# The diagonal of a linear attention by row products and the matrix engine, and the last output tile stored by thirds

## The chip, the cores and the metric

The kernel runs on one core of a Trainium2 chip. The metric is the time of one execution on the device in microseconds, lower is better. A core has a matrix engine (TensorE, PE in the rows; its weight loads are PEld), a vector engine (DVE), a scalar engine (ACT), GpSimd (POOL) and a sync engine (SP) that here only issues transfers. Each engine works through its own instructions in order and waits on semaphores. All numbers are float32 or its rounded form fp32r.

## What is computed

Three stages: a linear attention with decay over 4 sequences of 768 tokens and 8 heads of 48 features, then two feed-forward blocks over the 3072 tokens. The change is in how the first stage's diagonal term is made, and in how the last result is stored.

```python
for t in range(S):                                     # S = 768, head_dim D = 48
    cur = einsum('bhd,bhe->bhde', u * k[t], v[t])      # the diagonal term: token t sees itself, weighted by u
    y[t] = einsum('bhd,bhde->bhe', r[t], state + cur)
    state = w * state + einsum('bhd,bhe->bhde', k[t], v[t])
h = x @ w_in;  x = (max(h, 0) + alpha * min(h, 0)) @ w_out      # 384 -> 2048 -> 384
h = x @ w_in2; x = (h * tanh(softplus(h))) @ w_out2             # 384 -> 2048 -> 384
```

The diagonal term needs one number for each token and head: the sum over d of u[h, d] * r[t, h, d] * k[t, h, d].

## The kernel before

Tokens are cut into 24 chunks of 128. A chunk's attention is two units (four heads, or two pairs of heads, each); unit v belongs to chunk v // 2. For a unit, scaled keys and queries are made by POOL and DVE (`scale_key_level`, L320, and `scale_query_level`, L310), PE makes the scores level by level (`score`, L1092), ACT first writes the diagonal into `scores` (`fill_diagonal`, L865, an identity scaled by the token's number) and then copies the high levels over it (`copy_high`, L877), DVE picks the low levels under a mask (`pick_scores`, L605), and PE multiplies by the values (`attend`, L1118). `sum_state` (L1070) makes the state that the next chunk sees; ACT copies it out of PSUM (L863).

The feed-forward blocks take tiles of 512 tokens. Up and down products run over 16 steps (`up`, L1031, `down`, L1052); each step is nine matmuls of 512 columns, because weights and activations are split into a high and a low part. The attention of chunks 5 to 23 is spread over the steps of the first block. Chunks 0 to 4 have nothing to be hidden behind: this is the attention-only stage (`first_tile` of each engine), from the start to about 62 us. There PE also runs `warm` matmuls (L1021), which multiply the identity by itself into `acc[2]`. After unit 9 three more follow, and then the first `up`, which needs all that chunks 0 to 3 left in `x_parts`.

The inputs r and k arrive twice: `rk_rows` (from `rk_t`, one head feature in a partition, four pairs of heads by 128 tokens along the free axis; `load_rows`, L343) and `rkv_tok` (from `rkv`, one token in a partition, 384 features; `load_rk`, L351). The diagonal of a chunk is made from the latter: POOL multiplies r by k (`products`, L482), then by u (L486), DVE sums each head's 48 features (`sum_diagonal`, L629), and ACT's `fill_diagonal` waits for that at the chunk's first unit. In POOL's order of the stage a chunk has queries of unit 0, `rows_for_state` (L469) of the chunk before, `scale_for_state` (L496), queries of unit 1, `rows_for_state`, and `products` of the next chunk. After chunk 4 POOL splits weight slot 0 (L475).

SP issues, in its own order: decay, u (`bonus_tok`), rows, r and k, v of chunks 0 and 1, then for each chunk c its rows (which wait for the scores and state rows that still use the buffer), r and k of chunk c + 1, the holes of chunk c - 3 and v. Six heads' outputs fill 96 of 128 partitions of `x_parts`; the other two heads are copied into the holes by six small transfers for each chunk (`fill_holes`, L330). Of chunk 3's six, ACT issues three and SP three; SP's stand behind `load_weights(3)`, which waits for POOL's split of slot 0.

The last output tile: PE ends its last step, ACT copies the three banks `acc[0..2]` scaled by 2 (`copy_out`, L847) and issues one store of 768 KB.

## Time and profile before

| | |
|---|---|
| three timed runs, us | 980.93, 983.01, 983.13; median 983.01 |
| profiled execution, us | 983.2, of which the profile's span is 981.4 |
| busy share of the span | PE 98%, DVE 68%, ACT 63%, POOL 38% |
| PE busy by 40th of the span | 6 9 8 9, then 9 to the end, last 7 |
| granted PE clock by 40th | 7, then 9 |

Times in rows are microseconds from the span's start. "Idle before" and the name behind the arrow tell how long an engine had nothing in work and what let it go on; "issue" is time for which the profile shows no wait. The granted clock is 1.00 at 2.4 GHz and 0.50 at 1.2 GHz. PE's matmuls are pipelined and their ends modelled, so the distance from one start to the next is the better measure there.

### The profile page before, as it was taken

What the parts mean: (1) busy time and instruction counts of PE and PEld (TensorE: products, weight loads), DVE (VectorE), ACT (ScalarE), POOL (GpSimd) and SP (SyncE); (2) the same over time, 40 slices, a digit from 0 to 9 for tenths busy, and PEclk for the clock granted to TensorE, in tenths of its full rate; (3) what the DMA queues carried; (4) which work ended last, traced back from release to release, by engine and by line L of the source; (5) the groups of instructions that cost most, each with busy time, mean ns of one, the idle gap of its engine ahead of it and who ended that gap; (6) DMA issues with size and microseconds to landing.
All of it is one profiled execution on the core that took longest, in us unless ns stands there. A gap on an engine that the chain in (4) does not pass through costs nothing.

```text
span 981.4 us, 24146 instructions
## 1 busy us (share of the span) xinstructions
PE 964.2 (98%) x9568; PEld 786.5 (80%) x9568; DVE 664.7 (68%) x1384; ACT 622.7 (63%) x1285; POOL 373.2 (38%) x664
## 2 busy tenths in 40 slices
PE   6989999999999999999999999999999999999997
PEld 5668787888888888888888888888888888888886
DVE  7997776666666666556653437867777777677775
ACT  7766545454544455555445658878777777787775
POOL 8988787666666676666501430000000000000000
PEclk7999999999999999999999999999999999999999
DMA  6353322212211121111004230100001000000000
GB/s 187 100 151 107 111 64 78 56 49 59 78 48 59 48 78 45 46 54 55 15 10 173 97 115 33 33 12 21 33 33 33 0 32 0 22 10 1 33 0 33
DMA packets 22309, 54.33 MB, mean 55 GB/s; under 512 B 4928, under 2 KB 10432, under 8 KB 22208
## 3 DMA queue, kind: packets, MB, share of 16 engines
q1 hardware_dynamic: 20384, 43.43, 14.8%
q10 hardware_dynamic: 1824, 9.49, 2.4%
q8 instruction: 71, 1.16, 0.5%
q14 instruction: 30, 0.25, 0.1%
HBM read 41.10 MB, written 9.44 MB: 51 GB/s over the span
## 4 chain that ended last, share of the span: by engine, by line
PE 93%; POOL 5%; issue 1%; DMA 0%; ACT 0%; SPq 0%; POOLq 0%; ACTq 0%
PE acc L1063 41%; PE hid L1047 30%; PE lev L1047 10%; PE lev L1114 7%; POOL arena L317 2%; PE tok L1131 2%; PE tok L1137 2%; PE tok L1088 1%; POOL arena L469 1%; POOL ruk L482 1%; POOL arena L496 0%; POOL mask L448 0%; POOL ruk L486 0%; DMA x_parts<-y 0%; POOL w_lo L475 0%
## 5 line engine op out<-in xcount | busy, mean ns | idle before, releaser
L1047 PE MATMUL hid<-x_parts,w_hi 128*128 128x512 f32 x864 | 290.1, 390 | 1.6 <-DMA x_parts<-y 1.6
L1063 PE MATMUL acc<-g_hi,w_hi 128*128 128x512 f32 x576 | 231.3, 402 | 1.4 <-issue 1.4
L1063 PE MATMUL acc<-g_hi,w_lo 128*128 128x512 f32 x576 | 225.4, 391 | 0.0
L1047 PEld LDWEIGHTS hid<-x_parts,w_hi 128*128 128x128 f32 x864 | 162.4, 188 | 37.0 <-issue 2.7
L622 DVE COPY_PREDICATED scores<-mask,lev 64x128 f32<-64x128 int8 x420 | 149.9, 357 | 30.5 <-ACT scores L886 18.6
L1047 PE MATMUL hid<-x_parts,w_lo 128*128 128x512 f32 x432 | 168.3, 390 | 0.0
L1063 PE MATMUL acc<-g_lo,w_hi 128*128 128x512 f32 x576 | 163.0, 391 | 0.0
L931 ACT ACTIVATE relu_neg<-hid 128x512 f32<-128x512 f32 x96 | 57.2, 596 | 160.8 <-PE hid L1047 158.9
L709 DVE SCALAR_TENSOR_TENSOR hid<-relu_neg,neg_slope,hid 128x512 f32<-128x512 f32 x96 | 72.5, 755 | 124.7 <-ACT hid L932 124.3
L1063 PEld LDWEIGHTS acc<-g_hi,w_hi 128*128 128x128 f32 x576 | 108.2, 188 | 25.6 <-issue 2.0
L1063 PEld LDWEIGHTS acc<-g_lo,w_hi 128*128 128x128 f32 x576 | 108.5, 188 | 23.4 <-issue 0.3
L1063 PEld LDWEIGHTS acc<-g_hi,w_lo 128*128 128x128 f32 x576 | 108.3, 188 | 21.1
L317 POOL TENSOR_TENSOR arena<-arena,power 112x128 f32<-112x128 f32 x282 | 114.4, 440 | 18.3 <-DVE w_lo L703 18.3
L758 DVE SCALAR_TENSOR_TENSOR arena<-arena 128x512 f32<-128x512 f32 x96 | 66.4, 692 | 52.1 <-ACT arena L971 52.1
L845 ACT ACTIVATE g_hi<-hid 128x512 fp32r<-128x512 f32 x96 | 57.4, 598 | 68.5 <-DVE hid L709 67.7
L327 POOL TENSOR_TENSOR arena<-arena,power_rev 112x128 f32<-112x128 f32 x228 | 94.0, 447 | 16.3 <-PE lev L1114 15.0
L469 POOL TENSOR_TENSOR arena<-arena,power_split 112x512 f32<-112x512 f32 x46 | 58.7, 1277 | 99.9 <-PE tok L1137 99.9
L1047 PE MATMUL lev<-x_parts,w_hi 128*128 128x512 f32 x288 | 96.3, 389 | 0.0
L1047 PEld LDWEIGHTS hid<-x_parts,w_lo 128*128 128x128 f32 x432 | 81.2, 188 | 17.1
L693 DVE TENSOR_TENSOR g_lo<-hid,g_hi 128x512 fp32r<-128x512 f32 x96 | 66.2, 690 | 39.4 <-ACT g_hi L845 39.3
L1114 PEld LDWEIGHTS lev<-arena 48*64 48x64 f32 x4472 | 75.0, 136 | 11.1 <-issue 8.9
L1114 PE MATMUL lev<-arena 48*64 48x32 f32 (+1 forms) x4472 | 79.7, 223 | 2.5 <-DVE arena L317 1.8
(101 smaller groups left out, 1353.1 us busy)
## 6 DMA issues: line engine op xcount, KB each, us to landing
w_raw<-weights SPq DMA_DIRECT2D x32, 384.0 KB, 3.5
arena<-rk_t SPq DMA_DIRECT2D x48, 192.0 KB, 3.6
arena<-rkv SPq DMA_DIRECT2D x24, 384.0 KB, 3.2
arena<-rkv SPq DMA_DIRECT2D x24, 192.0 KB, 2.6
x_dram<-result ACTq DMA_DIRECT2D x6, 768.0 KB, 4.1
arena<-x_dram SPq DMA_DIRECT2D x6, 768.0 KB, 4.4
out<-result ACTq DMA_DIRECT2D x6, 768.0 KB, 3.3
x_parts<-y SPq DMA_DIRECT2D x141, 16.0 KB, 1.9
```

What stands on the lines that cost most here:

```text
L317: return engine.tensor_tensor(dst, src, spread(table[0:ROWS, pairs, 0:m], 2, CHUNK // (2 * m)), ALU.mult)
L327: return engine.tensor_tensor(dst, src, spread(table[0:ROWS, pairs, HALF - m:HALF], 2, CHUNK // (2 * m)), ALU.mult)
L469: nc.gpsimd.tensor_tensor(r_state[0:ROWS, x], spread(rk_rows[0:ROWS, par, 0, pairs], 1, 2), power_split[0:ROWS, :, pairs], ALU.mult).then_ ...
L622: nc.vector.copy_predicated(dst, pick, src).then_inc(pick_done if done < 2 * low_levels(rep) - 1 else mask_done, 1)
L693: nc.vector.tensor_tensor(g_lo[:, j % RING], hid[j % 2][:, 0:TILE], g_hi[:, j % RING].bitcast(F32), ALU.subtract).then_inc(glo_done, 1)
L709: nc.vector.scalar_tensor_tensor(hid[j % 2][:, 0:TILE], relu_neg[:, j % 2], neg_slope[:, j:j + 1], hid[j % 2][:, 0:TILE], ALU.mult, ALU.ad ...
L758: nc.vector.scalar_tensor_tensor(root[:, d], eps[:, d], 0.75, seed[:, d], ALU.add, ALU.mult).then_inc(root_done, 1)
L845: nc.scalar.activation(g_hi[:, j % RING], hid[j % 2][:, 0:TILE], ACT.Copy).then_inc(ghi_done, 1)
L931: nc.scalar.activation(relu_neg[:, j % 2], hid[j % 2][:, 0:TILE], ACT.Relu, scale=-1.0)
L1047: last = nc.tensor.matmul(to[:, 0:TILE], w[:, j, kt * P:(kt + 1) * P], x[:, par, kt], start=x is x_hi and w is w_hi and kt == 0, stop=x is ...
L1063: last = nc.tensor.matmul(acc[d][:, 0:TILE], w[:, j, cols], g[:, j % RING], start=j == 0 and g is g_hi and w is w_hi, stop=j == STEPS - 1 ...
L1114: last = nc.tensor.matmul(level_scores(banks, l)[tokens, 2 * q + u], k[rows, tokens], t[rows, wanted], start=True, stop=True)
```

## The change

For chunks 0 to 4 the diagonal is made in another way. POOL multiplies r by k once, in the row layout, into `rk_prod` (112 partitions by 512, double buffered in the memory of `relu_neg`, which this stage doesn't use). PE multiplies that by `u_rows`, a small new input that holds u in the columns of its head: for each of the four pairs of heads one matmul with the 112 by 128 product as weights and two columns moving, into the first eight columns of `acc[2]`. ACT copies these into `diag`. DVE's reduction goes for these chunks. From chunk 5 on all is as it was. The `warm` matmuls, which write the same bank, now wait for ACT's copy. The order on PE: chunk 0's diagonal ahead of unit 0's scores, the next chunk's behind each odd unit's `warm`.

The wide load of u moves from the head of SP's order to behind `load_weights(2)`; the small one stands behind the rows of chunk 0. r is no longer loaded by token for chunks 0 to 4.

At the end, the last down step runs output third by output third, three matmuls each, instead of all high parts and then all low parts. ACT copies and stores thirds 0 and 2, DVE copies third 1 and SP stores it: three stores of 256 KB.

```diff
+        rk_prod = relu_neg.rearrange("p r (a t) -> p r a t", a=PAIRS)
+        by_token = CHUNKS_PER_TILE + 1
# SP
             def load_rk(c):
-                reached(sp, s_rk, c - 1)
+                reached(sp, s_rk, c - 1 - by_token)
                 reached(sp, kstate_done, c - 1)
-                sp.dma_start(rkv_tok[:, c % 2, 0:2], rkv[c, :, 0:2]).then_inc(rk_in[c % 2], 16)
+                first = 0 if c >= by_token else 1
+                sp.dma_start(rkv_tok[:, c % 2, first:2], rkv[c, :, first:2]).then_inc(rk_in[c % 2], 16)
...
-            sp.dma_start(bonus_tok[:], bonus.partition_broadcast(P)).then_inc(s_bonus, 16)
             sp.wait_ge(zero_pool, 1)
             load_rows(0)
+            sp.dma_start(u_rows[0:ROWS], bonus_rows).then_inc(u_in, 16)
...
                 if c == 2:
                     load_weights(2)
+                    sp.dma_start(bonus_tok[:], bonus.partition_broadcast(P)).then_inc(s_bonus, 16)
...
-            sp.wait_ge(stored, 16 * 2 * TILES)
+            sp.wait_ge(last_copied[1], 1)
+            sp.dma_start(out[TILES - 1][:, 1], result[:, 1]).then_inc(stored, 16)
+            sp.wait_ge(stored, 16 * (2 * TILES - 1 + KT))
# POOL
+            def product_by_row(c):
+
+                pool.wait_ge(rows_in[c % 2], 32 * (c // 2 + 1))
+                reached(pool, diag_done, c - 1)
+                nc.gpsimd.tensor_tensor(rk_prod[0:ROWS, c % 2], rk_rows[0:ROWS, c % 2, 0], rk_rows[0:ROWS, c % 2, 1],
+                                        ALU.mult).then_inc(prod_in, 1)
...
-                products(1, 1, 1)
+                product_by_row(1)
...
-                    products(c + 1, 1 - par, (c + 1) // 2 + 1)
+                    if c + 1 < by_token:
+                        product_by_row(c + 1)
+                    else:
+                        products(c + 1, 1 - par, (c + 1) // 2 + 1)
...
-            products(0, 0, 1)
+            product_by_row(0)
# DVE
-                sum_diagonal(0, 0)
...
-                        sum_diagonal(c + 1, (c + 1) % 2)
+                        if c + 1 == by_token:
+                            sum_diagonal(c + 1, (c + 1) % 2)
...
+            dve.wait_ge(stored, 16 * (2 * TILES - 1))
+            dve.wait_ge(last_product, 2)
+            nc.vector.tensor_scalar(result[:, 1], acc[1][:, 0:TILE], 2.0, 0.0, ALU.mult, ALU.add).then_inc(last_copied[1], 1)
# ACT
+            def copy_diagonal(c):
+
+                act.wait_ge(diag_done, c + 1)
+                nc.scalar.activation(diag[:, c % 2], acc[2][:, 0:H], ACT.Copy).then_inc(s_diag, 1)
...
                     if x == 0:
+                        copy_diagonal(c)
                         fill_diagonal(v)
...
-            copy_out(2 * TILES - 1, out[TILES - 1], 2.0)
+            m = 2 * TILES - 1
+            act.wait_ge(stored, 16 * m)
+            for d in (0, 2):
+                act.wait_ge(last_product, d + 1)
+                nc.scalar.activation(result[:, d], acc[d][:, 0:TILE], ACT.Copy, scale=2.0).then_inc(last_copied[d], 1)
+                act.wait_ge(last_copied[d], 1)
+                act.dma_start(out[TILES - 1][:, d], result[:, d]).then_inc(stored, 16)
# PE
+            def diagonal(c):
+
+                pe.wait_ge(prod_in, c + 1)
+                reached(pe, s_diag, c)
+                for p in range(PAIRS):
+                    last = nc.tensor.matmul(acc[2][:, 2 * p:2 * p + 2], rk_prod[0:ROWS, c % 2, p], u_rows[0:ROWS, p],
+                                            start=True, stop=True)
+                last.then_inc(diag_done, 1)
...
+                pe.wait_ge(u_in, 16)
+                diagonal(0)
                 pe.wait_ge(zero_act, 1)
...
                     if PER_CHUNK <= v < FIRST - 1:
+                        pe.wait_ge(s_diag, v // PER_CHUNK + 1)
                         warm(acc[2])
+                    if v % PER_CHUNK and v < FIRST - 1:
+                        diagonal(v // PER_CHUNK + 1)
...
-            for j in range(STEPS - LAG2, STEPS):
+            for j in range(STEPS - LAG2, STEPS - 1):
                 down2(2 * TILES - 1, (TILES - 1) * STEPS + j, j)
+
+            j = STEPS - 1
+            pe.wait_ge(ghi2_done, TILES * STEPS)
+            pe.wait_ge(glo2_done, TILES * STEPS)
+            for d in range(KT):
+                cols = slice(KT * P + d * P, KT * P + (d + 1) * P)
+                for w, g in ((w_hi, g_hi), (w_lo, g_hi), (w_hi, g_lo)):
+                    last = nc.tensor.matmul(acc[d][:, 0:TILE], w[:, j, cols], g[:, j % RING], start=False, stop=g is g_lo)
+                last.then_inc(last_product, 1)
```

## Rows read from the trace of the kernel before

**Rows 1.** The chain that ended last, around the first up: start, duration, what.

```profile
56.13 1.84 POOL w_lo L475
...
58.48 3.31 DMA x_parts<-y
...
61.92 2.31 PE hid L1047 x9
```

**Rows 2.** Timeline of POOL: start, duration, line and instruction, idle before.

```profile
3.57 4.04 POOL L448 TENSOR_SCALAR_AFFINE_SELECT mask<-mask 128x64 int8<-128x64 int8 x10
9.12 1.00 POOL L482 TENSOR_TENSOR ruk<-arena 128x384 f32<-128x384 f32 x1 [1.51 <-DMA arena<-rkv]
...
11.16 2.41 POOL L317 TENSOR_TENSOR arena<-arena,power 112x128 f32<-112x128 f32 x6
...
33.66 1.01 POOL L482 TENSOR_TENSOR ruk<-arena 128x384 f32<-128x384 f32 x1
...
35.70 2.43 POOL L317 TENSOR_TENSOR arena<-arena,power 112x128 f32<-112x128 f32 x6
...
42.66 1.28 POOL L469 TENSOR_TENSOR arena<-arena,power_split 112x512 f32<-112x512 f32 x1
43.88 1.01 POOL L482 TENSOR_TENSOR ruk<-arena 128x384 f32<-128x384 f32 x1
```

**Rows 3.** Timeline of DVE, first pick and a whole chunk.

```profile
15.27 3.15 DVE L622 COPY_PREDICATED scores<-mask,lev 64x128 f32<-64x128 int8 x8 [1.11 <-ACT scores L886]
...
40.82 0.54 DVE L629 TENSOR_REDUCE diag<-ruk 128x8 f32<-128x384 f32 x1
41.28 3.17 DVE L622 COPY_PREDICATED scores<-mask,hid 64x128 f32<-64x128 int8 x8
...
50.73 0.54 DVE L629 TENSOR_REDUCE diag<-ruk 128x8 f32<-128x384 f32 x1
```

**Rows 4.** Timeline of PE in the stage: transposes, warm, units 0 to 4, unit 6.

```profile
7.09 0.65 PE L1028 MATMUL acc<-ident,power_rev 128*128 128x128 f32 x4 [0.49 <-DVE w_pow L587]
7.58 1.46 PE L1021 MATMUL acc<-ident 128*128 128x512 f32 x4
10.82 1.82 PE L1114 MATMUL lev<-arena 48*64 48x64 f32 x104 [1.78 <-DVE arena L317]
13.72 3.20 PE L1114 MATMUL hid<-arena 48*64 48x64 f32 x104 [1.08 <-POOL arena L317]
...
19.59 3.20 PE L1114 MATMUL lev<-arena 48*64 48x64 f32 x104
...
27.50 1.82 PE L1114 MATMUL hid<-arena 48*64 48x64 f32 x104
...
31.32 1.82 PE L1114 MATMUL lev<-arena 48*64 48x64 f32 x104
...
40.34 1.83 PE L1114 MATMUL lev<-arena 48*64 48x64 f32 x104 [0.23 <-issue]
```

**Rows 5.** PE in the windows of the clock's fall and rise: length, busy (count), granted clock, DMA.

```profile
13.00:14.00 1.00, 0.28 (x10) 0.82 0.18 48
...
27.00:28.00 1.00, 1.00 (x42) 0.85 0.00 0
```

**Rows 6.** Weight loads of `warm` on PE: ns min/median/max, first and last start.

```profile
L1021 PEld LDWEIGHTS acc<-ident x22: 186/189/337, 3.7 to 53.2; 128*128 128x128 f32 x22
```

**Rows 7.** Timeline of ACT, the first fill of the diagonal.

```profile
11.88 1.28 ACT L874 ACTIVATE scores<-ident,diag 128x128 f32<-128x128 f32 x4 [1.85 <-DVE diag L629]
```

**Rows 8.** The chain at the end: the copies ahead of the last store.

```profile
976.11 1.57 ACT result L855 x3
```

**Rows 9.** The page's list of transfers: KB each, median us from issue to landing.

```profile
arena<-rkv SPq DMA_DIRECT2D x24, 192.0 KB, 2.6
...
out<-result ACTq DMA_DIRECT2D x6, 768.0 KB, 3.3
```

**Rows 10.** Timeline of PE in the first block, where it once stood still.

```profile
119.23 0.63 PE L1063 MATMUL acc<-g_hi,w_hi 128*128 128x512 f32 x1 [1.37 <-issue]
```

23 lines of the change are left out of this document (18 added, 5 removed).

## The prediction

> **What bounds the kernel now.** The page says 98% PE, and from the first `up` at 61.92 to the last product PE hardly stops. The change touches only what lies ahead of that and the last store, so I read four things: who releases the first `up`, what the engines of the attention-only stage do, at what clock PE runs there, and the tail.
>
> The chain of waits at the first `up` reads backwards: the last holes, issued from 58.48, landed 3.31 later; ahead of them in SP's order is the load of weight slot 3, which waited for POOL's split of slot 0 (56.13 + 1.84) [rows 1]. Behind that stands POOL's order of the stage, without a pause from 9.12 on. One chunk on POOL lasts from 33.66 to 43.88, that is 10.2 us (its products start on the same beat; the reduction on DVE, 40.82 to 50.73, has a beat of 9.9) [rows 2, 3]. PE's beat of a whole chunk, unit 4 to unit 6, is 40.34 - 31.32 = 9.02 us, 0.23 of it a wait, so 8.8 of work [rows 4]. So three engines lie within 1.4 us of each other: whoever takes work off POOL and DVE and puts it on PE has to ask PE first.
>
> In its early part the stage runs at two clocks. The granted clock falls from 1.00 to 0.50 within 13 to 14 and is back within 27 to 28 [rows 5]; a unit's scores last 3.20 us in between and 1.82 outside [rows 4]. Before the fall PE had done one unit and nothing else since the warm matmuls ended at 9.04, with pauses of 1.78 and 1.08 [rows 4].
>
> **POOL.** For a chunk the two products take 35.70 - 33.66 = 2.04 us; the row product has 112 by 512 elements like `rows_for_state`, 1.28 by its row [rows 2]. It saves 0.76 for each of chunks 0 to 4. Chunk 0's also starts when the masks end (3.57 + 4.04 = 7.61) and not at 9.12, since it needs the rows and not the token load [rows 2]. POOL's first queries then begin at 8.9 where they began at 11.16: 2.3 us. Up to the split, four more chunks give 3.1: POOL alone would be 5.4 us early. Beat: 10.2 - 0.8 = 9.4.
>
> **DVE** loses a reduction for each chunk, 41.28 - 40.82 = 0.46: 9.9 becomes 9.45 [rows 3].
>
> **PE** gains, for each chunk, four matmuls in float32. They show as eight records (each float32 matmul of the trace has two, its transposes one), each with a load of 128 columns and two columns moving. Nearest row: the four transposes with their 128-column loads go by in 7.58 - 7.09 = 0.49, 0.12 each [rows 4]. Eight of them are 1.0 us; less the columns that don't move, I take 0.9. Ends: 0.5, if loads overlap as in the state sums, and 1.5, at the 188 ns that one load is shown with [rows 6]. At the half clock, double. PE's beat becomes 8.8 + 0.9 = 9.7: PE is now the longest of the three, and the chunk's gain is 10.2 - 9.7 at most, 0.2 against DVE's 9.9.
> The Trainium skill ("TensorE: Matmul & The Clock Gate", LDWEIGHTS (loading the stationary operand)) speaks against this use: a load costs by its columns, whatever the rows, columns / 1.2 ns. By it the eight loads are an estimated 0.85 us for two useful columns each, and the beat the same 9.65 us; the transposes' row agrees.
>
> **ACT** copies 128 by 8 out of PSUM for each chunk, about 0.25 us by the size of its small copies; in the steady part it has waited for DVE's sum, so this costs nothing while that slack stands (if it doesn't, 5 x 0.25). The copy waits for PE's diagonal and ACT's first copy of high scores is queued behind it. In chunk 0, the first fill began at 11.88 after an idle 1.85 for DVE's sum [rows 7]. Now: POOL's product ends at 8.9, PE is free of warms at 9.04, diagonal 9.95, copy and fill to 11.6; the scores of unit 0 run behind the diagonal, 9.95 to 11.75, and no longer start at 10.82.
>
> **SP.** The wide load of u (0.43 us of issue, 192 KB) no longer stands ahead of the rows of chunk 0, so these land about 1 us earlier than the 8.1 at which DVE began; that ceases to bind, as PE is held by the diagonal anyway. Behind `load_weights(2)` the moved load is followed by v of chunk 2, which waits for later work. The small load of u is needed at 9.0. One new need: POOL's row product of chunk 3 wants rows it formerly needed 2 us later, and these are loaded only after unit 3's scores. I reckon a stop of 0.6 us there, on POOL, which has room for it under PE.
>
> **The stage, worked down in order of time.** Unit 0's scores end at 11.75. High copies, weight split and fill follow on ACT as before: DVE's first pick starts at 13.7 (before 15.27 [rows 3]), and its second 2.1 earlier than before. Unit 2's scores start at about 17.9, before 19.59. From there to unit 3 the trace needed 27.50 - 19.59 = 7.9 us at the half clock [rows 4]: unit 3 at 25.8. If the clock still rises where it did, that unit's scores lose another 0.7. Three chunks of 9.7 follow to unit 9: 25.8 + 0.7 + 29.1 = 55.6. Before, the same three took 28.25 from 27.50, so 55.75: nearly the whole lead is spent on PE. Behind it some 0.5 is won, as SP's last holes don't wait for POOL's split any more. So with the slow stretch as it is, the stage ends 0.6 us early.
> But the stretch need not be as it is. Both first units now follow each other with no pause (9.95 to 13.5), and the first pause comes at about 15, where PE waits for the first pick; and the first `warm` inside the stretch comes 1.6 us earlier. I take 2 us less of half clock, worth half of it, 1 us. Ends: none, or 3.5 us less (1.8). **Stage: -1.6 us.**
>
> **Tail.** PE's last step has the same nine matmuls, so it ends at the same moment. Before, three copies in a row end at 976.11 + 1.57 = 977.68 [rows 8], because the last matmul of each bank came late. Now only the last bank's copy is left behind PE, 976.5 to 977.1: 0.6 earlier. The store behind it is 256 KB and not 768. Rows: 192 KB land in 2.6, 768 in 3.3 [rows 9]; in between lies 2.65, less 0.1 for other stores beside it: 0.6 to 0.7, with the bytes' own time saying more. **Tail: -1.3**, ends -0.5 (three completions in each other's way) and -1.9.
> The Trainium skill ("DMA: Bandwidth & Descriptors", Anatomy of one DMA) gives, for transfers issued by GpSimd, 2.0 us and then bytes at 436 GB/s: an estimate of 3.8 us for the whole store and 2.6 for a third, a difference of 1.2 and a tail of -1.8. The trace has 3.3 for the whole, so the rule's slope is not confirmed here.
>
> **Sum.** 983.2 (profiled execution, 0.2 over the median of 983.01) - 1.6 - 1.3 = **980.3**. A difference of 0.3%, 2.95 us, is about what can be told from none: faster begins at 980.06.
>
> **Rivals.**
> *PE keeps the high clock* (0.20). No pause between the units, and a diagonal beside them, speak for it; against it, units of scores fill little of the array, and only with warms did the clock come back. Unit 2 to unit 3 then takes about 4.5 and not 7.9; DVE and ACT bound that part, and the stage is 4.2 us early: 983.2 - 4.2 - 1.3 = 977.7.
> The Trainium skill (the same TensorE page, Part 1: The HAM clock gate) says that the half clock is the default and activity releases it; by it this rival holds if the diagonals count as activity, which no row shows.
> *The stop on PE's supply goes* (0.08). Once in the first block PE stood still for 1.37 with no wait shown, and the matmul behind it is shown with 0.63 us [rows 10]: the half clock had followed. New instructions ahead of it may move it away: 1.37 and, as an estimate, as much again and a little for the clock, 3.1 less, 977.2. It may as well double: that is the mirror, 983.4 (0.04).
> *Dear diagonals* (0.18), the other side. The eight loads don't overlap with anything: 1.3 to 1.5 us, double in the slow stretch, and the clock comes back some 3 us later. By the beat: 3 x 0.5 and 1.7 more than forecast, 983.5; it becomes slower by more than 0.3% where a diagonal costs 2 us (beat 10.8, stage +4.6, 986.5). Of the 0.18 a third lies there.
> *The edit doesn't do what it says* is a part of the forecast: POOL is relieved by 5.4 us and the stage by 1.6, since POOL was not alone.
>
> **Chances.** Forecast 0.50, from 978.9 to 982.0, with two fifths of it under 980.06. High clock 0.20 and the vanished stop 0.08 are faster; dear diagonals 0.12 same, 0.06 slower; mirror 0.04 mostly slower where diagonals are dear too. Faster 0.48, same 0.43, slower 0.09. Range 976.8 to 983.8: the high clock and most of the dear case are in it.
>
> **What the profile should show.** POOL's first queries near 8.9 and idle time later, behind PE. PE's diagonals of 0.9 us, a beat of 9.7, no waits for DVE's keys. The granted clock falls later than within 13 to 14 and rises before 27. First `up` near 60.3 (61.92 before); the tail from PE's end to the span's end 3.6 and not 4.9. Wrong would be: diagonals over 1.3, a slow stretch of the old length or none, a first `up` later than 61.9, or a last store that lands over 3 us after its issue.

## The result, and the profile after

The changed kernel takes 986.33 us (median of 11 runs, 984.11 to 990.37); the kernel before, beside it on the same chip, 981.72 (11 runs, 980.21 to 985.82). The ratio is 1.0047, 95% interval 1.0033 to 1.0061: 4.6 us slower. The forecast was 980.3 with a range of 976.8 to 983.8, so it went the other way, and the time lies outside the range.

The profiled execution of the changed kernel took 990.37 us, the slowest of the eleven, against 983.2 before. Of its 7.2 us more, 6.9 lie inside the profile's span, in three places: the first `up` starts 4.4 later (66.34 for 61.92), the stretch from there to the last product is 3.3 longer (917.5 for 914.2), and the tail, from the start of the last product to the end of the span, is 0.8 shorter (4.52 for 5.31).

| | before | after |
|---|---|---|
| unit 0, unit 2, unit 3 start (us) | 10.8, 19.6, 27.5 | 10.9, 19.2, 29.3 |
| unit 4 to unit 6, unit 6 to unit 8 | 9.0, 9.9 | 9.5, 9.5 |
| unit 8 to unit 9, unit 9 to first `up` | 5.5, 6.2 | 7.9, 5.2 |
| first `up` | 61.9 | 66.3 |
| low clock before the first `up`, in all | 13.7 | 17.1 |
| tail | 5.3 | 4.5 |

First PE, which has the answer. Timeline of PE in the changed kernel, start of the stage (start, duration, line and instruction, count, idle before and what ended it); the rows answer to [rows 4]:

```profile
8.00 2.23 PE L1060 MATMUL acc<-ident 128*128 128x512 f32 x4
10.06 0.95 PE L1185 MATMUL acc<-u_rows,relu_neg 112*128 112x2 f32 x8
10.94 1.82 PE L1153 MATMUL lev<-arena 48*64 48x64 f32 x104
12.60 1.79 PE L1153 MATMUL hid<-arena 48*64 48x64 f32 x98
15.24 0.31 PE L1153 MATMUL hid<-arena 48*64 48x32 f32 x6 [0.85 <-issue]
...
16.09 1.64 PE L1185 MATMUL acc<-u_rows,relu_neg 112*128 112x2 f32 x8
18.17 1.09 PE L1176 MATMUL tok<-scores,arena 128*48 128x128 f32 x8 [0.44 <-DVE scores L644]
19.19 2.77 PE L1153 MATMUL lev<-arena 48*64 48x64 f32 x88
23.77 0.65 PE L1153 MATMUL lev<-arena 48*64 48x32 f32 x16 [1.80 <-issue]
```

A unit's scores are 104 matmuls in one run. Units 1 and 2 are each cut in two, after 98 and after 88 of them, and the rest comes after 0.85 and 1.80 us in which PE waited for nothing that the trace shows. Later in the stage (same columns) the matmul group that sums the state is cut as well, and unit 9:

```profile
41.81 0.95 PE L1185 MATMUL acc<-u_rows,relu_neg 112*128 112x2 f32 x8
42.69 0.43 PE L1170 MATMUL tok<-arena,state 112*48 112x128 f32 x4
...
57.06 0.26 PE L1123 MATMUL tok<-state,result 112*64 112x48 f32 x3 [1.20 <-issue]
...
63.20 0.30 PE L1153 MATMUL acc<-arena 48*64 48x32 f32 x3 [0.29 <-issue]
...
66.34 0.47 PE L1086 MATMUL hid<-x_parts,w_hi 128*128 128x512 f32 x1
```

The four stops are 4.1 us together, nearly as much as the delay of the first `up`. The diagonal itself is what was foreseen: 42.69 - 41.81 = 0.88 us.

The windows of the whole stage, before and after, set this against what was won (window; length; busy and count for PE, PE's weight loads, DVE, ACT, POOL; granted clock; DMA share; GB/s):

```profile
9.00:61.95 52.95, 46.20 (x1318) 35.37 (x1317) 46.36 (x151) 36.31 (x128) 52.36 (x86) 0.87 0.49 136
```

```profile
9.00:66.40 57.40, 52.74 (x1361) 41.41 (x1359) 41.55 (x139) 36.65 (x131) 47.24 (x80) 0.85 0.41 110
```

POOL and DVE have each lost some 5 us of work, as meant. PE's busy time rose by 6.5: five diagonals of 0.88 and 0.7 more for the one at the half clock are 5.1, and 3.4 us more of low clock, at half the speed, 1.7. Its idle time fell only from 6.75 to 4.66. The idle time also changed its cause. Before, the four longest waits of PE were for DVE's keys (1.78), for the last holes ahead of the first `up` (1.6), for POOL's queries (1.08) and for DVE's pick (0.62); four more of 0.23 to 0.49 are marked "issue". After, in total (engine, line, releaser: us in total, times, longest):

```profile
PE lev L1153 <- issue: 1.8, 1, 1.8
PE tok L1123 <- issue: 1.2, 1, 1.2
PE hid L1153 <- issue: 0.9, 1, 0.9
PE tok L1176 <- DVE scores L644: 0.4, 1, 0.4
```

The waits for POOL, for DVE's keys and for the last holes, 4.5 us, are gone. They were the room in which the diagonals should have fitted. So PE is idle for less time than before, not for more: the stage is longer because PE's busy time grew by 6.5 us, and 4.1 of the idle time that is left are stops.

The fast part of the stage shows how little room there was (same columns; before, then after):

```profile
31.00:54.00 23.00, 21.79 (x698) 16.54 (x694) 21.43 (x69) 16.91 (x62) 22.84 (x39) 1.00 0.47 126
```

```profile
31.00:54.00 23.00, 23.00 (x675) 18.76 (x668) 19.90 (x65) 17.70 (x65) 22.28 (x40) 1.00 0.48 118
```

PE was 95% busy beside a POOL at 99%; now it is at 100%, and passes fewer matmul records in the same 23 us, 675 for 698, although eight of each chunk's are now the diagonal's.

POOL's own timeline bears out its part of the forecast: the row product at 7.59, the first queries at 8.82 (11.16 in [rows 2]). But then POOL idles behind PE:

```profile
7.59 1.27 POOL L505 TENSOR_TENSOR relu_neg<-arena 112x512 f32<-112x512 f32 x1
8.82 2.41 POOL L326 TENSOR_TENSOR arena<-arena,power 112x128 f32<-112x128 f32 x6
...
24.59 2.42 POOL L326 TENSOR_TENSOR arena<-arena,power 112x128 f32<-112x128 f32 x6 [2.75 <-PE lev L1153]
...
35.95 1.27 POOL L505 TENSOR_TENSOR relu_neg<-arena 112x512 f32<-112x512 f32 x1 [0.32 <-DMA arena<-rk_t]
```

### The profile page after: what moved, and what is told of

Its sections match the earlier page's. It is cut to its first block, busy times and chain, and to the rows that moved or that the text cites. A ratio compares the mean times of both kernels' runs of the same rounds, so it can differ in the third digit from the quotient of the medians.

```text
span 988.3 us, 24221 instructions
## 1 busy us (share of the span) xinstructions
PE 972.4 (98%) x9608; PEld 794.4 (80%) x9608; DVE 662.9 (67%) x1380; ACT 623.5 (63%) x1289; POOL 368.5 (37%) x659
## 3 DMA queue, kind: packets, MB, share of 16 engines
q8 instruction: 71, 1.16, 0.5%
## 4 chain that ended last, share of the span: by engine, by line
PE 90%; POOL 5%; issue 3%; DVE 1%; DMA 0%; ACT 0%; SPq 0%; POOLq 0%; DVEq 0%
PE acc L1102 39%; PE hid L1086 28%; PE lev L1086 10%; PE lev L1153 7%; PE tok L1176 2%; PE tok L1170 2%; POOL arena L326 2%; POOL arena L336 1%; PE tok L1127 1%; POOL arena L482 1%; PE acc L1060 1%; POOL w_lo L488 1%; DMA arena<-rk_t 0%; POOL arena L516 0%; PE hid L1153 0%
## 5 line engine op out<-in xcount | busy, mean ns | idle before, releaser
L482 POOL TENSOR_TENSOR arena<-arena,power_split 112x512 f32<-112x512 f32 x46 | 58.8, 1277 | 107.9 <-PE tok L1176 105.0
L336 POOL TENSOR_TENSOR arena<-arena,power_rev 112x128 f32<-112x128 f32 x228 | 92.5, 441 | 17.1 <-PE lev L1153 15.5
L1086 PEld LDWEIGHTS hid<-x_parts,w_lo 128*128 128x128 f32 x432 | 81.2, 188 | 17.1
L1153 PEld LDWEIGHTS lev<-arena 48*64 48x64 f32 x4472 | 76.0, 137 | 10.1 <-issue 10.1
```

The lines of the kernel that those rows point to most:

```text
L336: return engine.tensor_tensor(dst, src, spread(table[0:ROWS, pairs, HALF - m:HALF], 2, CHUNK // (2 * m)), ALU.mult)
L482: nc.gpsimd.tensor_tensor(r_state[0:ROWS, x], spread(rk_rows[0:ROWS, par, 0, pairs], 1, 2), power_split[0:ROWS, :, pairs], ALU.mult).then_ ...
L1086: last = nc.tensor.matmul(to[:, 0:TILE], w[:, j, kt * P:(kt + 1) * P], x[:, par, kt], start=x is x_hi and w is w_hi and kt == 0, stop=x is ...
L1153: last = nc.tensor.matmul(level_scores(banks, l)[tokens, 2 * q + u], k[rows, tokens], t[rows, wanted], start=True, stop=True)
```

## What a stop marked "issue" is

The profile has DMA queues of the kind "instruction". The page after counts the loads of queue 8 (queue and kind: packets, MB, share), 1.16 MB in 71 loads, 16 KB each:

```profile
q8 instruction: 71, 1.16, 0.5%
```

I numbered PE's records in the order of the trace (matmuls, weight loads, and the waits and jumps of its sequencer, which are 267 of 19483 in the changed kernel) and wrote down at which number each stop lies and when the load of queue 8 before it ran. The twelve profiles have thirty stops up to 145 us with no releaser and a load directly ahead of them. All lie, to within one record, at the numbers 450, 706, 1474, 1730, 2498, 2754, 3778, 4290 and 4546: multiples of 256 apart. The reading: these are PE's instructions, and when PE enters a block of 256, the load of the next one is asked for. Not every row marked "issue" is such a stop. The four of 0.23 to 0.49 us of the kernel before (at 40.3, 45.9, 50.2 and 55.7) and the one of 1.65 at 134.3 in the changed kernel lie on no edge of a block. The numbers read from the traces, in us (the fourth column is the start of the last instruction ahead of the edge):

```
kernel, line of the stop     enters    load begins, ends    at the next      goes on   from load's end
                             a block                        block's edge
changed, L1153               12.11     12.69   13.84        14.17            15.24     1.40
changed, L1153               15.24     21.33   22.31        21.67            23.76     1.45
late u, same place           14.46     19.18   20.12        21.15            21.67     1.55 (0.22 idle)
changed, L1123               53.23     54.79   55.74        55.65            57.06     1.32
before, L1063                111.99    116.84  117.93       117.47           119.23    1.31
tail only, L1077             111.61    115.88  116.96       117.31           118.36    1.40
last warms split, L1128      107.91    116.44  117.53       116.76           119.03    1.50
```

Of the eighteen loads of the changed kernel up to 136 us, ten begin 0.5 to 1.1 us after PE entered the block, three sooner and five later. They take 0.9 to 1.4, and PE goes on 1.3 to 1.5 after the load's end if it had to wait (up to 1.7 in the other kernels). So some 3.3 us must pass between two edges, by an estimate from these three. A unit of scores is 208 instructions in 1.75 us at the high clock, and where the edge falls behind such a unit PE is there too early. Worse is a load that begins late. In the changed kernel nothing of queue 8 moved from 15.3 to 21.3. The queues of those 6 us (queue and kind: packets, MB, share; then the issues: KB each, median us to landing):

```profile
q1 hardware_dynamic: 659, 1.46, 85.6%
...
arena<-rk_t SPq DMA_DIRECT2D x2, 192.0 KB, 3.5
w_raw<-weights SPq DMA_DIRECT2D x1, 384.0 KB, 4.2
arena<-rkv SPq DMA_DIRECT2D x1, 192.0 KB, 3.3
bonus_tok<-bonus SPq DMA_DIRECT2D x1, 192.0 KB, 4.2
```

The load of PE's instructions began at 21.33, when the data of SP's queue, 86% of what the engines can move, had gone by. The last of these five loads is `bonus_tok`, which the change moved there.

Data in the way is not the only reason for a late load. Behind the stop at 57.06 PE entered its next block, and the load began at 60.59, 3.5 us later, with nothing to stand behind (window; columns as above):

```profile
57.10:60.50 3.40, 3.40 (x20) 1.79 (x21) 0.04 (x1) 0.33 (x1) 1.66 (x1) 0.53 0.02 5
```

The stop of 0.29 at 63.20 is the end of that block. The kernel before has the same behind its stop at 119.23 (load at 122.65), the kernel with 13 small warms behind 105.94 (load at 111.09), both at a DMA share of 0.02 or less. What holds these loads up is open.

That is a reading so far. The experiments test it against the plainer one, that the diagonals are simply more work on PE.

## The experiments

Each was timed beside the kernel before on the same chip, whose median was 982.19 (the first four), 982.61 (the next four) and 981.80 (the last two). In one table, with the readings from each profile (us):

```
kernel            median   ratio to before          first up  unit 0 to  low clock  first 16  tail
                                                              first up   in stage   steps
before            981.72   -                        61.9      51.1       13.7       88.8      5.3
changed           986.33   1.0047 (1.0033-1.0061)   66.3      55.4       17.1       92.2      4.5
tail only         980.49   0.9982 (0.9971-0.9993)   61.8      51.1       10.2       88.1      3.6
stage only        988.04   1.0059 (1.0042-1.0076)   66.4      55.8       20.5       89.0      5.3
one pair          982.12   0.9995 (0.9983-1.0007)   60.1      49.8       10.2       90.4      4.6
matmuls only      985.00   1.0029 (1.0017-1.0041)   62.9      52.4       13.3       87.4      5.3
13 small warms    990.24   1.0072 (1.0045-1.0099)   72.2      59.4       34.6*      90.2      4.5
45 small warms    990.37   1.0088 (1.0070-1.0106)   70.8      53.9       23.9       87.3      4.5
late u            986.22   1.0040 (1.0024-1.0056)   64.1      54.2       17.1       89.7      4.5
fewer warms       984.96   1.0029 (1.0013-1.0045)   67.6      56.5       27.3       88.4      4.5
warms split       981.02   0.9991 (0.9978-1.0004)   61.4      50.9       13.7       89.9      3.7
late u, split     986.78   1.0049 (1.0031-1.0067)   64.0      54.0       17.1       91.5      4.5
* 27.8 us of them by the durations of the matmuls, since this run's record of the clock begins only at 35.9 us
```

### The two halves alone

The tail of the change on the kernel before, and the stage of the change with the old tail.

```diff
# tail only: the kernel before, plus
+            m = 2 * TILES - 1
+            act.wait_ge(stored, 16 * m)
+            for d in (0, 2):
...
+                act.dma_start(out[TILES - 1][:, d], result[:, d]).then_inc(stored, 16)
# stage only: the changed kernel, minus the same lines
```

> The kernel before with the new tail alone (last step by thirds, three stores). Theory A (the stage lost the time, the tail is a small gain): 0.8 to 1.3 us faster than before, since in the profile of the changed kernel the last matmul starts 4.5 us ahead of the span's end where it was 5.3. Rival: the three stores and the copy on DVE get in each other's way in most executions, then it is level or up to 1 us slower.

> The changed kernel with the old tail. Theory A: all of the loss lies in the stage, so this is slower than before by 4.6 + 1 = 5 to 6 us. Rival (the tail is at fault): level with before or faster. In the profile theory A wants stops of PE with no wait shown, each ending 1.3 to 1.5 us behind the end of an instruction load; the profile of the changed kernel has them at 14.2 to 15.2, 21.7 to 23.8 and 55.7 to 57.1.

Measured: 980.49 and 988.04, so the tail wins 1.7 us and the stage alone costs 5.9. The sum, 4.2, is about what both together cost (4.6, interval 3.2 to 6.0). The loss is all in the stage. In the profile of the stage-only kernel the first `up` is at 66.37, and the stops are there, at the same instructions as in the changed kernel:

```profile
15.25 0.31 PE L1141 MATMUL hid<-arena 48*64 48x32 f32 x6 [1.23 <-issue]
...
22.84 0.65 PE L1141 MATMUL lev<-arena 48*64 48x32 f32 x16 [0.80 <-issue]
...
56.99 0.34 PE L1111 MATMUL tok<-state,result 112*64 112x48 f32 x3 [1.96 <-issue]
```

The place is constant, the length is not: it depends on when the load begins. The tail-only kernel is faster than the kernel before by 0.18% (0.07 to 0.29), and so than the changed one by about 0.65%.

### Less work on PE, and PE's work alone

One pair: the changed kernel with one of the four diagonal matmuls of each chunk; it leaves out the diagonal of the other three pairs of heads. Matmuls only: the kernel before, with four matmuls of the diagonal's shape in the diagonal's five places, on POOL, DVE and ACT nothing changed.

```diff
# one pair
-                for p in range(PAIRS):
+                for p in range(1):
# matmuls only: the kernel before, plus, called ahead of unit 0 and where the change calls diagonal()
+            def diagonal():
+                for p in range(PAIRS):
+                    nc.tensor.matmul(acc[2][:, 2 * p:2 * p + 2], power[0:ROWS, p], ident[0:ROWS, 0:2],
+                                     start=True, stop=True)
```

> The changed kernel in which PE makes the diagonal of the first pair of heads alone (one matmul of four for each chunk; the other heads' diagonal is left out). POOL's and DVE's relief stays, PE has 12 instructions and 0.67 us less a chunk. Theory B (PE's beat of 9.7 was the price): five chunks give 3 x 0.67 = 2 us, so slower than before by 2.5. Theory C (PE runs out of instructions because two units' scores follow each other at the full clock and the loads of instructions queue behind SP's data): the stop near 14 and the one near 22 stay, the one at 56 goes or moves; slower than before by 1 to 3. If neither, and the relief of POOL and DVE is worth what the forecast said: 3 us faster than before.

> The kernel before with the twenty matmuls of the diagonals added to PE at the same places, on other operands and used by nobody; POOL, DVE, ACT and SP are as before. Theory B: PE's work of a chunk goes from 8.8 to 9.7 and stays under the beat of 10.2, so 0 to 1 us slower than before. Theory C: the blocks in which PE's instructions are loaded shift by 16 for each chunk, so that stops may appear in chunks 3 and 4, 1 to 2 us each; but the first two units are not brought together, so the stop near 14 isn't there. 1 to 3 us slower.

Measured: with one pair 982.12, the same as before; the other three pairs are worth 4.2 us by the medians (986.33 - 982.12) and 5.1 by the ratios (1.0047 and 0.9995), each taken beside the kernel before. The matmuls alone, with nothing relieved, cost 2.8. So it is PE's part of the change that loses. POOL's relief shows no gain in the medians: the one-pair kernel has the whole of it, a quarter of the diagonals, and the tail's 1.7 besides, and only reaches the time of before. In its profile the first `up` is 1.8 us earlier than before (60.08), and the first sixteen steps, with a stop of 2.02 at 118.23, are 1.6 longer. The profile of the matmuls-only kernel is of an execution at 982.68, among the fastest of its twelve, and does not show where the 2.8 of the medians lie.

How much of this is work and how much is stops? From unit 0 to the first `up` the one-pair profile has 49.8 us and the changed one 55.4, 5.6 more. Stops of the one-pair kernel:

```profile
14.99 0.67 PE L1127 MATMUL tok<-arena 128*64 128x48 f32 x16 [1.24 <-issue]
...
22.30 0.42 PE L1153 MATMUL lev<-arena 48*64 48x32 f32 x4 [0.56 <-issue]
```

1.8 us, and the later ones are missing: the changed kernel has 4.1 - 1.8 = 2.3 us more of them. But the one-pair kernel waits for other things instead, 1.54 for DVE's pick, 0.75 for the last holes and 0.39 marked "issue" at 49.5. Its window of the whole stage, to be held against that of the changed kernel above (52.74 busy in 57.40):

```profile
9.00:60.10 51.10, 46.40 (x1331) 35.95 (x1329) 41.77 (x139) 36.19 (x129) 47.01 (x80) 0.90 0.43 121
```

PE is idle for 4.70 us in one and 4.66 in the other. The whole difference is in its busy time: three quarters of the diagonals, 24 x 0.11 = 2.6 for the four chunks behind unit 0 and 0.5 more for the chunk at the half clock, and the clock itself, low for 17.1 us against 10.2, which by half of it is 3.4. (The 0.5 is in both.) So the stops' own time does not come out as a loss between these two; what does is the diagonals' work and the half clock, about half each, and one stretch of the latter, from 57.3 to 60.7, stands behind a stop.

The matmuls-only kernel had neither of the two early stops, but one of 1.08 us at 53.95 and one of 0.91 at 59.06, on the edges 2498 and 2754; its diagonals are the same eight records of 0.95. That a kernel without the relief has fewer stops than one with it fits the reading: with POOL slower PE enters its blocks later.

### Other instructions at the edges

Two kernels put more instructions ahead of the stage: 13 small matmuls in place of the last two `warm`, 44 instructions more in the trace, and 45 of them, 172 more.

```diff
-            for n in (PAIRS, PAIRS // 2):
-                warm(acc[2], n)
+            for _ in range(13):   # the other kernel: 45
+                nc.tensor.matmul(acc[2][0:HALF, 0:32], ident[0:D, 0:HALF], ident[0:D, 0:32], start=True, stop=True)
             first_tile()
```

> The changed kernel in which the second group of warm matmuls (8 instructions) is replaced by 13 small ones (48 by 64 weights, 32 columns; 52 instructions), so that everything behind stands 44 instructions later in PE's program. Control of the next run. Theory C (PE's instructions come in blocks of 256; the next block is asked for when the one before it is entered and takes 3 us or more; the profile of the changed kernel has its stops at PE's instructions 450, 706, 2498 and 2754 of the trace): the boundaries move 44 instructions back in the program, the stop of unit 1 stays, one of 0.8 appears in chunk 3: 3 to 6 us slower than before, as the changed kernel. Rival D (the stops belong to fixed waits or to the clock, not to the place in the program): the stops stay where they were, same time as the changed kernel.

> The same with 45 small matmuls (180 instructions), 172 later than in the changed kernel. Theory C: taking the distances between instructions from the profile of the changed kernel, no block of 256 between the start and the first up is used up in under 3.3 us any more, so all stops of the stage go: 1 to 3 us faster than before (the stage's first up near 60 and the tail's 1.8), though the 45 matmuls cost 1.5 to 2.5 us where there were 2.2 of warm ones. Rival D: as f1_shift13, 3 to 6 us slower than before.

Measured: 990.24 and 990.37. As a cure both failed, since two `warm` are not to be had cheaper: unit 0 starts at 12.8 and at 16.9 instead of 10.9, and PE is at the half clock until 35.9 and 35.3 us, with 13 from the first diagonal on, with 45 from 11.4. In the kernel with 13 only the durations show it: its record of the clock begins at 35.9 us, and a window ahead of that prints 1.00 because nothing is recorded there (a window of it, and the diagonal and unit 0 in its timeline):

```profile
14.00:20.00 6.00, 6.00 (x191) 5.84 (x185) 3.08 (x11) 4.21 (x15) 3.80 (x9) 1.00 0.19 68
```

```profile
10.98 1.86 PE L1185 MATMUL acc<-u_rows,relu_neg 112*128 112x2 f32 x8
12.78 3.20 PE L1153 MATMUL lev<-arena 48*64 48x64 f32 x104
```

That the early stops are gone in both says therefore little about the place: at the half clock a unit's 208 instructions take 3.0 us, and PE no longer outruns its loads. The part at the high clock says more. With 13 the stop at instruction 2498 is there, and longer, in the first sum after the scores of unit 8 (56.87):

```profile
60.97 0.24 PE L1123 MATMUL tok<-state,result 112*64 112x48 f32 x1 [2.03 <-issue]
```

With 45 this one is gone, and one appears in the same kind of place two chunks earlier, behind the scores of unit 4 (39.68), at instruction 1474, where no other kernel had one (the one with fewer warms has 0.69 us at the next edge, 1730):

```profile
43.15 0.26 PE L1123 MATMUL tok<-state,result 112*64 112x48 f32 x2 [1.46 <-issue]
```

So the stop does not belong to a step of the work, nor to a dependency of the sum: it moves through the program as instructions are put ahead of it, and stays on the edges of the blocks. What was expected of 45 small warms, a stage without a stop, failed: the load ahead of this edge began 2.4 us after PE had entered the block, at a DMA share of 0.95.

### The wide load of u one chunk later

```diff
                     load_weights(2)
-                    sp.dma_start(bonus_tok[:], bonus.partition_broadcast(P)).then_inc(s_bonus, 16)
                 if c > 2:
                     fill_holes(sp, c - 3)
+                if c == 3:
+                    sp.dma_start(bonus_tok[:], bonus.partition_broadcast(P)).then_inc(s_bonus, 16)
                 load_v(c)
```

> The changed kernel with the wide load of u one chunk later in SP's order. If the stop near 22 comes from PE's instruction load standing behind SP's data (asked for at 15.2, begun at 21.3), it is the last 192 KB of these that are taken away: the load begins 0.5 to 0.8 us earlier, and the kernel is 0.5 to 1 us faster than the changed one (4.6 slower than before), so 4 slower than before. If the queue is not the cause: no difference.

Measured: 986.22, ratio 1.0040 (1.0024 to 1.0056). The load of PE's instructions begins at 19.18 instead of 21.33, right behind a shorter run of data, and the stop of 1.80 is one of 0.22:

```profile
18.67 2.77 PE L1154 MATMUL lev<-arena 48*64 48x64 f32 x88
21.67 0.66 PE L1154 MATMUL lev<-arena 48*64 48x32 f32 x16 [0.22 <-issue]
```

The other profiles show how much of this may be the move. Where the wide load stands as the change puts it, PE's load at this edge began 6.1 (changed), 5.9 (fewer warms), 5.4 (stage only) and 4.9 us (one pair) after PE had entered the block, and the stop was 1.80, 1.25, 0.80 and 0.56. Where it stands a chunk later, PE's load began 4.7 (late u) and 4.4 us after (late u, split), and the stop was 0.22 and none. So the order fits, but the same order of loads alone gives a spread of 1.2 us, and one profile of each kernel cannot say that the whole 1.6 us is the move's.

The first `up` is 2.2 earlier in the profile, of which 1.0 is there at unit 0 already (9.96 for 10.94). In the medians, by the ratios, only 0.7 us is seen (1.0040 for 1.0047), and the two intervals overlap; the stops that end at 55.0 and 61.3 are there as before, 1.33 and 0.51 us.

### Fewer warm matmuls

PE is the bound, so take something off it: the `warm` of units 5 and 7 is left out.

```diff
-                    if PER_CHUNK <= v < FIRST - 1:
+                    if PER_CHUNK <= v < FIRST - 1 and (v % PER_CHUNK == 0 or v == 3):
```

> The changed kernel without the warm matmul of units 5 and 7, whose place the diagonal takes. Theory B (PE's work was the price): PE's beat falls from 9.7 to 8.6 in two chunks, 1 to 2 us faster than the changed kernel. Theory C: the same instructions in less time, so a block of 256 is used up sooner and the stops get longer; the time saved in the warms comes back as stops: within 1 us of the changed kernel, 4 to 5 slower than before.

Measured: 984.96 (983.02 to 991.12), 1.0029 to before, against 1.0047 of the changed kernel: perhaps 1.8 us better, but the intervals overlap. In its profiled execution, at 987.99 one of its longer ones, the granted clock was low for 27.3 us of the stage and not for 17.1; whether the missing `warm` brought that about, one profile does not show. It is no way out.

### The last warms in smaller pieces

Twelve `warm` matmuls of 128 columns instead of three of 512, at the end of the stage: the same columns, but more instructions, none of them ahead of anything in the stage. Once on the tail-only kernel, once on the late-u kernel.

```diff
-                for _ in range(3):
-                    warm(hid[1])
+                for _ in range(3 * PAIRS):
+                    warm(hid[1], 1)
```

> The kernel before with the new tail, and the three last warm groups of the attention-only stage (three products of 512 columns) written as twelve of 128 columns: the same columns, 18 more TensorE instructions, all behind the stage's work. Theory C (the stops marked issue are TensorE reaching a block of 256 instructions before its load is there; which instruction stands at a boundary decides whether it stops): the stage is unchanged (first up within 0.4 us of the tail-only kernel's 61.75), but the boundary that cost 1.05 us at 117.3 to 118.4, with the low clock from 118.5 to 121.9 behind it, now falls on other instructions of the same step; the stop goes or at least changes by over 0.3 us. If it goes with its low clock the kernel takes 978 to 979 us against the tail-only kernel's 980.5; if it only moves, 979.5 to 982. The rival, that the stop belongs to a place in the work (what the step waits for) and not to a count of instructions: stop and low clock stay at the same instruction of the step, and the time is that of the tail-only kernel, 980.5 within 0.5.

> The changed kernel with the wide copy of u loaded one chunk later in the order of the loads (986.2 us, ratio 1.0040 to before) and the three last warm groups of the stage written as twelve products of 128 columns, 18 more TensorE instructions behind the stage's work. Theory C: stops at 13.2, 53.4 and 60.6 us stay where they were, since they lie ahead of the split; from the boundary behind it on the stream stands elsewhere against the blocks, and the first sixteen steps, 89.7 us before, move by what stops there come or go, between 88.1 and 92. In all 984.5 to 988.5. The rival, that the count of instructions does not matter: 986.2 within 0.5, the first sixteen steps 89.7 within 0.3.

Measured: 981.02, ratio 0.9991 (0.9978 to 1.0004), and 986.78, 1.0049 (1.0031 to 1.0067): neither is better than the kernel that it was made from. (The expectations say 18 instructions more; in the trace, where a float32 matmul has two records and each its load, there are 36.) The hope of a version without the stop at 118 was wrong: it grew from 0.65 to 2.05 us. What the run was made to tell apart it does tell. In the tail-only kernel the stop was between two matmuls of a `down` step, in this one it is 16 matmuls before the end of the unit ahead of it, so 36 instructions earlier in the work; its number is 4290 in both (first tail only, then with the warms split):

```profile
117.31 0.40 PE L1077 MATMUL acc<-g_hi,w_lo 128*128 128x512 f32 x1
118.36 0.70 PE L1077 MATMUL acc<-g_hi,w_hi 128*128 128x512 f32 x1 [0.65 <-issue]
```

```profile
115.40 1.59 PE L1128 MATMUL lev<-arena 48*64 48x64 f32 x88
119.03 0.43 PE L1128 MATMUL lev<-arena 48*64 48x32 f32 x16 [2.05 <-issue]
```

PE entered the block before that one 3.7 us earlier than in the tail-only kernel, at 107.9, and this should have given the load time. It did not begin before 116.44: 8.5 us, of which the last five are SP's run of weights and rows (the engines' share is 0.81 to 1.07 from 111 to 116), while from 108 to 111 nothing moved at all. Why the load was not asked for in those three free microseconds, no row shows; in the late-u kernel, from an edge at 109.6, it took 0.87. The one-pair kernel is a second case: from an edge at 108.17, with the engines idle until 110.5, the load began at 115.80, and the stop at 118.23 is 2.02.

In both kernels the granted clock is low after the stop (windows of the tail-only kernel; columns as above):

```profile
118.00:119.00 1.00, 0.64 (x2) 0.55 (x3) 0.00 (x0) 1.00 (x4) 1.00 (x3) 0.75 0.00 0
119.00:120.00 1.00, 1.00 (x4) 0.81 (x3) 0.91 (x3) 0.74 (x4) 1.00 (x4) 0.50 0.00 0
```

From 118.5 to 121.9 PE works at 1.2 GHz: 3.4 us, half of it lost, more than the stop itself. The changed kernel has the same at 57.3 to 60.7, behind its stop at 57, with a `warm` of 2.08 us for two records that take 1.12 elsewhere. It is why unit 8 to unit 9 needs 7.9 us and before 5.5: 1.2 of stop, 1.7 of clock, less what the wait of 0.49 had been.

## Why the prediction was wrong, point by point

In short, the step that failed is the stage, put at -1.6 us, where the stage alone costs 5.9 in the medians and 4.4 in the profile. The sum gave PE 0.9 us a chunk for the diagonals and let the rest of its time stand as before; it had no term for the supply of PE's instructions in the stage (four stops, 4.1 us), and took the half clock 2 us shorter where it was 3.4 longer. Which part of the 5.9 belongs to which of these is not settled; that it comes with the diagonals on PE, the one-pair and the matmuls-only kernels show.

**Right: POOL, DVE, the diagonal.** The row product takes 1.27, the first queries start at 8.82 (8.9 was said), DVE's first pick at 14.86 (13.7 was said, 15.27 before; the missing 1.1 is the `warm` group, which in this execution ran at the half clock from 8.00 to 10.2 and held the first diagonal until 10.06. The tail-only kernel has this too, so the change did not bring it). A diagonal takes 0.88 (0.9), doubled in the slow stretch (16.09, 1.64). PE's beat from unit 4 to unit 6 is 9.51 (9.7). The Trainium skill's price of a weight load by its columns ("TensorE: Matmul & The Clock Gate", LDWEIGHTS) gave 0.85 and is borne out: eight loads of 128 columns pass in 0.88. ACT's copy is 0.18, and POOL's stop for rows of chunk 3 is there, 0.32 instead of 0.6. "Dear diagonals" was not the case.

**Wrong: unit 2 to unit 3 stays at 7.9.** It took 10.1. Unit 2 started at 19.2 (17.9 said), because unit 1 had lost 0.85 to a stop and the diagonal of the slow stretch stands between it and unit 2. Then came the stop of 1.80. The prediction had counted this stretch by the durations before, and asked of each engine only what it would do, not how its instructions come to it.

**Wrong: three chunks of 9.7 to unit 9, and 0.5 won behind it.** Unit 3 to unit 9 took 31.8 and not 29.1: 1.20 of stop and 1.7 of low clock behind it. Before, these chunks ran with PE at 95% and took 28.25 us, 9.4 each: above the 9.0 of unit 4 to unit 6 from which PE's work was read, and below POOL's 10.2. The room for 0.9 of diagonal was therefore smaller than the 1.4 us (10.2 - 8.8) that it was set against.

**Wrong in sign: a slow stretch 2 us shorter.** The clock fell later, between 16 and 17, as was said, but came back at 30.0 and not before 27: 13.6 us as before (13.7). With the second stretch behind the stop the stage has 17.1 us of it, 1.7 us lost where 1 was to be won. That the clock fell later was luck: in the tail-only kernel, which has no diagonal, it fell at 16.1. The rival of a high clock throughout did not happen in any of the profiles, with diagonals or without: all have 10 to 35 us of half clock in the stage. The rule that activity releases the clock (the same page of the Trainium skill, Part 1: The HAM clock gate) is consistent with this, but beside the diagonals, in the changed kernel, the clock fell all the same.

**The stage in one sum.** Forecast -1.6, profile +4.4, a miss of 6.0. The stops are 4.1 us. The clock, 1.7 lost for 1 won, is 2.7. Together 6.8, and other waits fell, those for POOL, DVE and the holes from 5.1 to 0.4. This sum is bookkeeping and not a division of the cause: against the one-pair kernel the stops' time was made up by other waits.

**The rival that was named and underrated.** The prediction knew the stop at 119 [rows 10], called it a stop on PE's supply, and gave 0.12 to its going or doubling. It took it as one event in the first block, with a price of 3 us at most, and did not ask why it was there. Its own evidence said so: the stop had no releaser, it stood behind a unit's scores, and a load of kind "instruction" ended 1.31 ahead of it. Read like this, the question for a change that puts 80 instructions more on PE (sixteen for each diagonal, loads counted) ahead of a chain that runs at 95% is where the edges will fall, and that no case of the prediction contained. Of the rivals on the slower side, dear diagonals had the right size (983.5 to 986.5) for the wrong reason.

**The tail: -1.3 forecast, -1.7 by the tail-only run.** Its end is 3.64 behind the last product's start, against 5.31: 1.67, and the Trainium skill's rule for a transfer ("DMA: Bandwidth & Descriptors", Anatomy of one DMA), by which the estimate was -1.8, comes closer here than the bound by rows, though by a difference of two figures that are each 0.5 too high: the stores of 256 KB land 2.1 us after their issue, where the rule gives 2.6 and the prediction took 2.65, and the whole of 768 KB landed in 3.3, where it gives 3.8. In the changed kernel the same tail wins only 0.8, and there it lands in 3.0. The difference is in the DMA of the tail (stores of the tail-only kernel, then of the changed kernel):

```profile
out<-result ACTq DMA_DIRECT2D x2, 256.0 KB, 2.1
out<-result SPq DMA_DIRECT2D x1, 256.0 KB, 2.1
```

```profile
q14 instruction: 1, 0.01, 0.4%
...
out<-result ACTq DMA_DIRECT2D x2, 256.0 KB, 3.0
out<-result SPq DMA_DIRECT2D x1, 256.0 KB, 2.5
```

In the changed kernel a load of instructions on queue 14, for some engine other than PE, runs from 985.19 to 985.50, while all three stores (issued at 983.55, 984.72 and 984.85) are under way; in the tail-only kernel and the one with split warms there is none at that time, and the tail is 3.6. All seven profiles with the new stage and the new tail have this load, and a tail of 4.5 to 4.6. That it delays the stores fits in all of them, but no run took it away, so it is not shown.

**The first block.** Of the profiled execution's 7.2 us, 3.3 are from the first `up` to the end, all in the first sixteen steps (92.2 for 88.8; the next sixteen take 92.0 and 92.2). There is a stop of 1.65 at 134.3, and this one is no supply stop: the matmul behind it reads the state that DVE had finished just before (L623, 133.43 with four of them). Behind it the clock is low from 135.8 to 142.7. In the stage-only kernel, with the same stage and a stop of 1.53 in the same place, the clock stayed high and these steps took 89.0. So the low clock is not a cost of the change but of that execution. The stop at this line is in seven of the twelve profiles, 1.28 to 1.65 us, and the other five have a supply stop between 118 and 129 us in its place.

**What stays open.** How the medians divide between the diagonals' work, the half clock and the stops is not known; no run has the diagonals and no stop. Why some loads of instructions began 3.4 to 8.5 us after PE had entered the block, with the DMA engines idle for the first two or three of these or for all of them, is not settled either.

## What to carry to other kernels

An engine at 95% beside the bounding one at 99% is not a place to put work: the relieved engine's time comes back as its idle time behind the other. Before adding many small matmuls to a stage, look for idle rows marked "issue" with an instruction load ending 1.3 to 1.5 us ahead of them, and for long runs of data transfers beside a burst of small matmuls (here six microseconds at a share of 86%); there an added instruction, or a transfer that nobody waits for, may cost time on PE. And a change in two parts should be timed in two parts: here one part is worth -1.7 us and the other +5.9, and the kernel to keep is the tail alone, 980.5.

## What the runs showed of the hardware that was not expected

- PE's instructions come in loads of 16 KB, one for each 256 of them, the sequencer's own counted (71 loads and 19483 records in the changed kernel). Most loads take 0.9 to 1.4 us, and PE goes on 1.3 to 1.7 us behind the end of one that it had to wait for. With 208 instructions in 1.75 us, PE outruns it.
- Such a load can come late. It began 6.1 us after PE had entered the block while SP's queue used 86% of the DMA engines, and 4.4 to 5.9 us after in five other profiles with nearly the same run of data. It also began 3.4 to 5.1 us late with the engines idle (at 57.07 in the changed kernel, 119.23 before, 105.94 with 13 small warms).
- A stop in an otherwise full stream can bring the half clock: of the nineteen stops of 1 us or more marked "issue" between 30 and 145 us of the twelve profiles, ten had the clock low within 2.1 us of their end, for 3.4 us in six and 6.8 in four, and nine did not (1.46 us at 43.15 with 45 small warms, for one, with the clock at 1.00 from 43 to 50).
- A record of the clock can begin late, and a window ahead of it prints 1.00: with 13 small matmuls in place of the last `warm`, units took 3.20 us and not 1.82 from 12.8 to 35.
- Three stores of 256 KB on two queues landed in 2.1 us each in the tail-only kernel, and in 2.5 to 3.0 in the changed one, with a load of another engine's instructions beside them.
